# Probabilities of sequences 1 to 3 transposed by VectorE blocks and DMAs through DRAM instead of TensorE, with new engine orders

## The reference

```python
# 1. attention with a sliding window of 64 (4 sequences, 8 heads, head size 64)
scores = scale * q @ k.T ; scores where not (0 <= i - j < 64) = -1e9
attn = exp(scores - max) ; attn = attn / (sum(attn) + 1e-9)
x = attn @ v                                  # -> (4, 576, 512)
# 2. gated MLP with a spatial (token) mixing
h = relu(x @ w_in) ; u, v = halves of h       # 512 each
v_s = einsum('ts,bsd->btd', w_spatial, layernorm(v)) + b_spatial
y = (u * v_s) @ w_out
# 3. mixer: over tokens, then over channels
h = relu(y.T @ w_tok1) @ w_tok2 ; u2 = y + h.T
out = u2 + relu(u2 @ w_ch1) @ w_ch2
```

## Time and profile before

| | |
|---|---|
| median of 3 runs | 691.25 us (691.11 to 691.32) |
| profiled execution, its own time | 691.28 us |
| span in the profile | 689.4 us |
| TensorE busy | 670.6 us, 97% of the span |
| TensorE's granted clock, mean | 0.997 |
| VectorE, ScalarE, GpSimd busy | 47%, 33%, 22% of the span |
| DMA engines busy | 29.8% on the one queue that SyncE issues |

### The profile page before, as it was taken

The page is one execution under the profiler, slowest core; times in us unless marked ns, Lnnn a source line. Parts: engine busy times, 40 slices in busy tenths (PEclk is TensorE's granted clock), DMA queues, the critical chain, the costliest instruction groups (busy, mean ns, idle before and its releaser), DMA issues.

```text
span 689.4 us, 11477 instructions
## 1 busy us (share of the span) xinstructions
PE 670.6 (97%) x4133; PEld 621.2 (90%) x4133; DVE 323.7 (47%) x893; ACT 229.5 (33%) x642; POOL 150.8 (22%) x237
## 2 busy tenths in 40 slices
...
DMA packets 139555, 50.66 MB, mean 73 GB/s; under 512 B 124145, under 2 KB 127793, under 8 KB 139505
## 3 DMA queue, kind: packets, MB, share of 16 engines
q1 hardware_dynamic: 139504, 50.00, 29.8%
...
## 4 chain that ended last, share of the span: by engine, by line
PE 92%; DVE 3%; issue 1%; DMA 1%; ACT 1%; POOL 1%; SPq 0%; DVEq 0%; ACTq 0%; POOLq 0%
PE ps L1123 68%; PE ps L1219 11%; PE ps L1188 5%; PE ps L1163 4%; PE ps L1173 2%; DMA att<-in_moe_w_ch_dram 1%; PE ps L1282 1%; DVE gate L1008 1%; PE ps L1142 1%; DVE arena L1014 1%; DVE att L907 0%; ACT att L700 0%; PE ps L1207 0%; DVE att L1111 0%; ACT arena L776 0%
## 5 line engine op out<-in xcount | busy, mean ns | idle before, releaser
L1123 PE MATMUL ps<-arena 128*128 128x288 f32 (+3 forms) x2064 | 354.5, 326 | 5.4 <-DVE att_r L1047 4.3
L1123 PEld LDWEIGHTS ps<-arena 128*128 128x128 f32 (+1 forms) x2064 | 324.8, 187 | 24.4 <-DVE att_r L1047 4.7
L1123 PE MATMUL ps<-arena,att_r 128*128 128x512 f32 x648 | 161.1, 393 | 0.0
L1047 DVE SCALAR_TENSOR_TENSOR att_r<-ps,att_r 128x384 fp32r<-128x384 f32 x72 | 39.9, 556 | 228.7 <-ACT att_r L810 228.7
L1123 PEld LDWEIGHTS ps<-arena,att_r 128*128 128x128 f32 x648 | 120.6, 188 | 22.0
L810 ACT ACTIVATE att_r<-ps 128x384 fp32r<-128x384 f32 x72 | 35.3, 491 | 241.8 <-PE ps L1123 241.8
L1219 PE MATMUL ps<-arena 128*128 128x288 f32 (+1 forms) x560 | 89.8, 316 | 0.0
L638 POOL TENSOR_SCALAR att<-att,rinv 128x128 f32<-128x128 f32 x144 | 55.8, 408 | 135.5 <-DVE rinv L918 135.3
L1219 PEld LDWEIGHTS ps<-arena 128*128 128x128 f32 x560 | 80.3, 188 | 3.9
L720 ACT ACTIVATE att<-att,nmax 128x128 f32<-128x128 f32 x144 | 55.9, 390 | 14.4 <-DVE nmax L907 14.3
L1188 PE MATMUL ps<-att 128*128 128x128 f32 x288 | 37.6, 276 | 3.3 <-DVE att L927 3.1
...
## 6 DMA issues: line engine op xcount, KB each, us to landing
u_scratch<-uy SPq DMA_DIRECT2D x16, 288.0 KB, 2.8
att<-u_rows SPq DMA_DIRECT2D x18, 256.0 KB, 5.0
out_dram<-att SPq DMA_DIRECT2D x18, 256.0 KB, 2.1
att<-in_v_dram SPq DMA_DIRECT2D x16, 256.0 KB, 3.7
att<-in_k_dram SPq DMA_DIRECT2D x48, 72.0 KB, 2.5
att<-in_q_dram SPq DMA_DIRECT2D x48, 72.0 KB, 2.8
u_rows<-early SPq DMA_DIRECT2D x48, 72.0 KB, 2.7
...
```

What stands on the lines that cost most here:

```text
L1047: dve.scalar_tensor_tensor(out=h3[:, j % RING, 1, :], in0=ps[:, 6 + j % 2, 0:CK], scalar=0.0, in1=h3[:, j % RING, 0, :].bitcast(F32), op0= ...
L1123: ins = pe.matmul(dst, w[a], x[c], start=first and n == 0, stop=last and n == 2, skip_group_check=True)
```

## The change

For sequences 1 to 3 the 27 `T` units of TensorE and the 27 `c` units of VectorE are gone. In their place VectorE turns the probabilities in 32 x 32 blocks from `prob` to `pT` (`pt`), in an order that makes a block-row of all four head pairs contiguous; one DMA (`pw`) stores the 256 KB to a scratch tensor in DRAM, and four DMAs (`pr`) of 64 KB bring them back with the block-rows and block-columns exchanged, into the same buffer `pT`. `V` then reads its moving operand as four pieces of 32 columns, 128 columns apart. Sequence 0 keeps the old way. `m` of a block waits for `pt` of three blocks earlier. `pt` waits for `V` of two blocks earlier. All lists of orders are new; those of POOL and the ACT and DVE lists of the earlier segments are left out below.

```diff
     FIRST_PE = (
-        "g00 + g10 + S0 S1 g20 + g30 + g01 + g11 + g21 + g31 S2 T0 S3 + y00 + y10 + y20 + y30 + y01 S4 V0 S5 T1 "
-        "t0 + y11 + T2 V1 t1 y21 + y31 + S6 T3 V2 a0 a1 t2 T4 V3 t3 S7 V4 t4 a2 a3 a4 T5 S8 T6 V5 v0 + V6 T7 b00 "
-        "b10 b20 b30 b01 b11 b21 b31 v1 V7 T8 + V8 v2 + v3 + v4 + u00 + u10 + u20 + u30 + u01 + u11 + u21 + u31 +").split()
+        "g00 + g10 + S0 S1 g20 + S2 g30 + g01 + g11 S3 + g21 + g31 + y00 + y10 + V0 S4 y20 V1 S5 + y30 + y01 + "
+        "y11 + y21 S6 V2 t0 t1 S7 + y31 + a0 V3 t2 a1 t3 V4 S8 t4 a2 a3 v0 a4 + V5 V6 b00 v1 + b10 b20 v2 + b30 "
+        "V7 V8 b01 b11 b21 b31 v3 + v4 + u00 + u10 + u20 + u30 + u01 + u11 + u21 + u31 +").split()
     LOOP_PE = (
-        "g00 S0 S1 + g10 + g20 + g30 + g01 + g11 + S2 T0 S3 T1 g21 + g31 V0 S4 S5 + y00 + y10 + T2 S6 V1 V2 y20 + "
-        "y30 + y01 + t0 T3 t1 T4 y11 + y21 + y31 + V3 S7 t2 T5 V4 t3 S8 t4 T6 V5 a0 a1 a2 a3 T7 a4 V6 V7 v0 + b00 "
-        "T8 b10 b20 V8 b30 v1 + b01 b11 b21 v2 + b31 v3 + v4 + u00 + u10 + u20 + u30 + u01 + u11 + u21 + u31 +").split()
+        "S0 S1 g00 + g10 S2 S3 + g20 + g30 + g01 + g11 + g21 + g31 + y00 + V0 S4 V1 S5 y10 + y20 + y30 + y01 + "
+        "y11 V2 t0 S6 V3 + y21 + y31 + S7 t1 t2 S8 V4 t3 t4 a0 a1 a2 a3 v0 a4 V5 V6 + v1 + b00 b10 b20 b30 b01 "
+        "b11 V7 V8 v2 + b21 b31 v3 + v4 + u00 + u10 + u20 + u30 + u01 + u11 + u21 + u31 +").split()
...
     LOOP_DVE = (
...
+        "qt0 qt1 qt2 m0 qt3 m1 qt4 r0 r1 m2 pt0 sa00 sm00 pt1 gl00 sa10 sm10 sa20 qt5 m3 sm20 gl10 sa30 gl20 sm30 "
+        "sa01 r2 gl30 sa11 sm01 r3 sm11 pt2 m4 gl01 pt3 sa21 gl11 sm21 sa31 sm31 gl21 vo1 gl31 r4 m5 qt6 pt4 r5 "
+        "m6 qt7 vo2 tl0 pt5 qt8 r6 tl1 tl2 vo3 pt6 m7 tl3 m8 r7 tl4 r8 al0 pt7 al1 pt8 vo4 te00 te10 vs0 te20 "
+        "te30 vs1 vn0 vl0 te01 te11 vn1 te21 te31 vl1 vs2 kt0 ut0 ut1 vn2 vs3 vl2 ut2 vs4 vn3 vn4 ut3 vl3 kt1 vl4").split()
...
     EPILOGUE_ACT = (
-        "gh00 gh10 gh20 wb0 gh30 wb1 gh01 wb2 gh11 wb3 yy00 gh21 wb4 gh31 yy10 wb5 yy20 wb6 yy30 yy01 th0 yy11 "
-        "th1 yy21 wb7 yy31 uf0 th2 wb8 th3 th4 ah0 ah1 wb9 H0 H1 wb10 wb11 wb12 wb13").split()
+        "wb0 gh00 wb1 wb2 gh10 gh20 gh30 gh01 gh11 wb3 gh21 gh31 yy00 yy10 yy20 wb4 yy30 wb5 yy01 th0 th1 yy11 "
+        "wb6 yy21 wb7 yy31 uf0 th2 th3 wb8 th4 ah0 ah1 wb9 wb10 wb11 H0 wb12 wb13 H1").split()
...
     ALL_SP = (
...
+        "lq00 lk00 lq01 lv00 lv01 lq02 lk01 lk02 lw00 lw01 lk03 lq03 lw02 lv02 lv03 lz04 lw04 lv04 lk10 lw06 lq10 "
+        "lw03 pw10 lv10 pw11 pr10 pr11 lw05 lv11 pw12 pw13 pr12 lv12 pr13 pw14 pr14 pw15 lv13 pw16 pr15 pr16 lv14 "
+        "pw17 pw18 pr17 pr18 lk20 st00 st01 st02 st03 lq20 sr00 sr01 sr02 sr03 pw20 pr20 pw21 lv20 lv21 pr21 pw22 "
+        "pw23 pr22 pr23 lv22 pw24 pr24 pw25 lv23 pw26 pr25 pr26 lv24 pw27 pw28 pr27 pr28 lk30 st10 st11 st12 st13 "
+        "lq30 sr10 sr11 sr12 sr13 pw30 pw31 pr30 pr31 lv30 pw32 lv31 pw33 pr32 pr33 lv32 pw34 pr34 pw35 lv33 pw36 "
+        "pr35 pr36 pw37 lv34 pw38 pr37 pr38 wb40 st20 sr20 st21 st22 sr21 st23 sr22 sr23 wb41 wb42 wb43 wb44 wb45 "
+        "wb46 wb47 uf40 wb48 wb49 wb410 wb411 wb412 wb413 st30 st31 sr30 sr31 sr32 sr33 st32 st33").split()
...
+        prob_dram = nc.dram_tensor("prob_blocks", (2, 4, P, P), F32, kind="Internal").ap()
...
+        def back_count(g):
+
+            return sum(n % 2 == g % 2 for n in range(BL, g + 1))
...
+                if kind == "pw":
+                    g = BL * b + x
+                    sp.wait_ge(prob_turned, PROB_TURNED["pt", b, x])
+                    sp.dma_start(prob_dram[g % 2].rearrange("j q n -> q j n"), pT[:, g % 2, :].rearrange("q (j n) -> q j n", j=4)) \
+                        .then_inc(prob_out_dram[g % 2], 16)
+                if kind == "pr":
+                    g = BL * b + x
+                    sp.wait_ge(prob_out_dram[g % 2], 16 * back_count(g))
+                    for j in range(4):
+                        sp.dma_start(pT[32 * j:32 * j + 32, g % 2, :].rearrange("c (i n) -> c i n", i=4),
+                                     prob_dram[g % 2, j].rearrange("(i c) n -> c i n", c=32)).then_inc(prob_back[g % 2], 16)
...
-                    dve.wait_ge(*use_full("T", b0, blk0))
+                    dve.wait_ge(*(use_full("T", b0, blk0) if b0 == 0 else (prob_turned, PROB_TURNED["pt", b0, blk0])))
...
+            def turn_prob(b, blk):
+
+                g = BL * b + blk
+                b0, blk0 = divmod(g - 2, BL)
+                dve.wait_ge(*use_full("V", b0, blk0))
+                apart(dve)
+                dve.wait_ge(prob_done, g + 1)
+                dve.transpose(pT[:, g % 2, :].rearrange("q (j p r) -> q p j r", j=4, p=PAIRS),
+                              prob[:, g % 3, :].rearrange("q (p j r) -> q p j r", p=PAIRS, j=4)).then_inc(prob_turned, 1)
...
-                pe.wait_ge(*use_free("T", b, blk))
+                if b == 0:
+                    pe.wait_ge(*use_free("T", b, blk))
+                    keys = pT[:, g % 2, :].rearrange("k (p n) -> k p n", p=PAIRS)
+                else:
+                    pe.wait_ge(prob_back[g % 2], 64 * back_count(g))
+                    keys = pT[:, g % 2, :].rearrange("k (i p r) -> k p i r", i=4, p=PAIRS)
                 for p in range(PAIRS):
                     ins = pe.matmul(tp[:, bank, P * p:P * (p + 1)], window[:, P * p:P * (p + 1)],
-                                    pT[:, g % 2, P * p:P * (p + 1)], start=True, stop=True)
+                                    keys[:, p], start=True, stop=True)
```

More of the change, by code:

```diff
@@ L57, in bass_attention_gmlp_mixer_kernel @@
     PROLOGUE_PE = (
-        "Q0 K0 Q1 S0 K1 S1 S2 K2 S3 Q2 T0 V0 S4 T1 S5 V1 T2 T3 V2 V3 T4 v0 T5 V4 V5 Q3 + K3 v1 + Z4 S6 S7 v2 S8 "
-        "w0 + u00 + u10 + T6 u20 T7 V6 w1 + T8 V7 u30 V8 w2 + v3 w3 w4 + v4 + u01 w5 + u11 + u21 + u31 +").split()
+        "Q0 K0 Q1 S0 S1 K1 K2 S2 Q2 S3 T0 T1 S4 V0 T2 V1 T3 K3 Q3 S5 V2 S6 V3 T4 w0 v0 w1 w2 V4 S7 T5 Z4 w3 + V5 "
+        "v1 + S8 T6 v2 + V6 T7 u00 w4 + u10 + T8 V7 u20 V8 + u30 + v3 + w5 v4 + u01 + u11 + u21 + u31 +").split()
     FIRST_PE = (
-        "g00 + g10 + S0 S1 g20 + g30 + g01 + g11 + g21 + g31 S2 T0 S3 + y00 + y10 + y20 + y30 + y01 S4 V0 S5 T1 "
@@ L68, in bass_attention_gmlp_mixer_kernel @@
+        "b11 V7 V8 v2 + b21 b31 v3 + v4 + u00 + u10 + u20 + u30 + u01 + u11 + u21 + u31 +").split()
     EPILOGUE_PE = (
-        "g00 + g10 + g20 + g30 + g01 + g11 + g21 + g31 + y00 + y10 + y20 + y30 + y01 + y11 + t0 t1 y21 + y31 + a0 "
-        "t2 a1 t3 t4 a2 a3 a4 H0 H1 b00 b10 b20 b30 b01 b11 b21 b31").split()
+        "g00 + g10 + g20 + g30 + g01 + g11 + g21 + g31 + y00 + y10 + y20 + y30 + y01 t0 t1 + y11 + y21 + y31 + a0 "
+        "t2 t3 a1 t4 a2 a3 a4 H0 b00 b10 b20 b30 b01 b11 b21 b31 H1").split()
@@ L71, in bass_attention_gmlp_mixer_kernel @@
     PROLOGUE_ACT = (
[L72 to L73 removed]
+        "qe0 qe1 e0 e1 qe2 e2 e3 o0 o1 e4 qe3 xh0 o2 e5 wh0 o3 wh1 xh1 o4 e6 vr0 o5 ze4 xh2 e7 wh2 vh0 vr1 wh3 e8 "
+        "wh4 o6 uu00 vr2 o7 xh3 o8 xh4 uu10 uu20 vh1 uu30 vr3 vh2 vr4 wh5 uu01 vh3 vh4 uu11 uu21 uu31").split()
     FIRST_ACT = (
[L75 removed]
@@ L76, in bass_attention_gmlp_mixer_kernel @@
-        "e5 o2 yy31 th2 e6 th3 th4 o3 e7 o4 ah0 ah1 o5 vr0 o6 e8 o7 vr1 vh0 o8 vr2 vh1 vh2 vr3 uu00 vr4 uu10 uu20 "
-        "vh3 vh4 uu30 uu01 uu11 uu21 uu31").split()
+        "gh00 e0 e1 gh10 gh20 e2 gh30 gh01 e3 gh11 o0 yy00 yy10 o1 gh21 gh31 yy20 e4 yy30 yy01 yy11 e5 th0 th1 "
+        "yy21 e6 yy31 th2 o2 th3 o3 th4 e7 e8 o4 ah0 ah1 vr0 o5 vr1 vh0 o6 o7 vr2 vh1 o8 vr3 vh2 vr4 uu00 uu10 "
+        "vh3 uu20 vh4 uu30 uu01 uu11 uu21 uu31").split()
     LOOP_ACT = (
-        "gh00 e0 gh10 e1 gh20 gh30 e2 e3 gh01 o0 e4 yy00 gh11 o1 gh21 o2 gh31 yy10 yy20 yy30 e5 yy01 th0 th1 yy11 "
@@ L80, in bass_attention_gmlp_mixer_kernel @@
-        "yy21 e6 yy31 o3 th2 o4 th3 th4 e7 e8 o5 ah0 ah1 o6 o7 vr0 o8 vr1 vh0 vh1 vr2 vh2 vr3 uu00 uu10 vr4 vh3 "
-        "uu20 vh4 uu30 uu01 uu11 uu21 uu31").split()
+        "e0 e1 gh00 e2 gh10 gh20 e3 gh30 yy00 o0 gh01 gh11 e4 yy10 gh21 gh31 yy20 yy30 o1 yy01 e5 th0 yy11 e6 "
+        "yy21 yy31 o2 th1 th2 th3 o3 th4 e7 e8 o4 ah0 ah1 o5 vr0 vr1 o6 o7 vh0 o8 vh1 vr2 vr3 vh2 vr4 uu00 uu10 "
+        "vh3 uu20 uu30 vh4 uu01 uu11 uu21 uu31").split()
     EPILOGUE_ACT = (
-        "gh00 gh10 gh20 wb0 gh30 wb1 gh01 wb2 gh11 wb3 yy00 gh21 wb4 gh31 yy10 wb5 yy20 wb6 yy30 yy01 th0 yy11 "
@@ L88, in bass_attention_gmlp_mixer_kernel @@
-        "wl1 vn2 xl4 wl2 kt1 wl3 vl2 wl4 vs3 vs4 vn3 wl5 vn4 vl3 vl4").split()
+        "ke0 m0 vo1 m1 ke1 r0 ke2 r1 m2 m3 hv0 hv1 r2 c0 c1 r3 m4 c2 hv2 hu0 c3 hu1 ke3 r4 m5 lv0 xl0 hv3 c4 vo2 "
+        "r5 lv2 wl0 m6 c5 m7 xl1 hu2 hu3 r6 wl1 vs0 xl2 vo3 vn0 r7 c6 m8 wl2 wl3 vl0 r8 vs1 c7 vo4 c8 vs2 wl4 xl3 "
+        "vn1 kt0 vn2 xl4 vl1 kt1 vl2 vs3 vs4 wl5 vn3 vn4 vl3 vl4").split()
     FIRST_DVE = (
[4 rows of a table removed]
-        "vs4 ut3 vn4 vl3 vl4 kt1").split()
[4 rows of a table added]
+        "vs4 vn3 ut2 vl3 ut3 vn4 kt0 vl4 kt1").split()
```

22 lines of the change are left out of this document (12 added, 10 removed), and 15 rows, old and new, of tables (ALL_SP, FIRST_DVE, LOOP_DVE).

## The result

| | before | after |
|---|---|---|
| median, run side by side | 691.25 us (691.11 to 691.32, 4 runs) | 671.91 us (671.60 to 672.14, 4 runs) |
| span of the profiled execution | 689.4 us | 670.2 us |

The ratio is 0.971, 95% interval 0.9697 to 0.9723: faster, by 2.9%. First the page of the kernel after, against the earlier trace rows: TensorE does 108 matmuls fewer, is busy 13.4 us less, and is idle for 13.0 us instead of 18.8.

What follows compares the result with a forecast made beforehand. TensorE was taken as the bound, busy 670.6 of 689.4 us. From 691.3, minus 11.9 (transposes), 4.3 (epilogue stall) and 0.5 (gate), plus 2 (`V` waits) and 2 (boundaries), gave 678.6 us, range 672 to 684.

Steps and rivals of the forecast that it cites:

- `T` removed: TensorE in sequences 1 to 3: dropping 27 transpose units of 0.44 us each saves 11.9 us in full.
- epilogue stall: Epilogue: TensorE's 4.28 us idle goes once wb410 to wb413 load ahead of `st30`; minus 4.3 us.
- gate: Epilogue: TensorE's gate wait of 1.1 us may go or grow; minus 0.5 us (minus 1.1 to plus 1.5).
- waits of `V`: Sequences 1 to 3: all waits of `V` together add 2 us (0 to 8).
- trip: `pt`, store to DRAM and reads back: 7.5 us per block, bounds 6.5 and 9.3, fitting everywhere by 1 to 3 us.
- boundaries: Both segment boundaries: q may load late for the next segment's first unit; plus 2 us together (0 to 6).
- prologue: Start of the kernel: same units in another order, still limited by the exponent chain; 0 us (minus 2 to plus 2).
- + 2 + 2: End of the forecast sum: 2 us for all waits of `V` plus 2 us for both segment boundaries.
- Given back: Rival for the whole kernel: the gain was nowhere or is given back exactly; 690 to 692.5 us, chance 0.04.
- slower: Rival: the DRAM round trip becomes the bound, near 702 us at an 11.5 us trip; chance 0.13, DRAM trip 0.10 of it.
- break-even: Sequences 1 to 3: the gain of 16.7 us is lost at a trip of 10.6 us, given mean slack of 1.7 us.
- Plain DMAs are the wrong tool: Rival on the store: if its pieces cost like 128-byte ones, the trip is 9.7 us, time 685; no separate chance.

## Why the prediction was too high

| step | predicted | measured | from |
|---|---|---|---|
| `T` removed, 27 x 0.44 | -11.9 | -11.7 busy; -11.4 with the waits | second stretch |
| epilogue stall | -4.3 | -5.7 | fourth stretch; half clock 1.40 |
| gate | -0.5 | -1.5 | third stretch |
| waits of `V` | +2 | +0.3 | waits; at most 0.6 without the trip |
| boundaries | +2 | 0 | S0 never idle behind q |
| prologue | 0 | -0.4 | first stretch |

All errors but small ones lie on one side. The differences are -1.4 (clock), -1.0 (gate), -1.7 (trip), -2 (boundaries), -0.4 (prologue) and small remainders, together the missing 6.5 us between 678.6 and the profiled 672.1.

**The mechanisms held, the sizes did not.** The transposes were on the bound and are saved in full: taken out, 11.7 us (the new epilogue with and without them); put back, 11.0. The strided operand is free (276 ns), `pt` costs 0.71 for 0.70. The stall came from the four weight loads behind `st30`: moving these alone removed it.

**The step that failed was a size in the sum.** The largest was its last line, "+ 2 + 2": 4 us for waits that the same text had shown to fit, everywhere, by 1 to 3 us. Its own lists gave 8.6 us of need against 9.6 of slot; a forecast of the likeliest case would have put 0 there and kept the 4 us for the upper bound. The measured total is 0.3. The trip was also overestimated, 7.5 against 6.7: I had put the last read at 2.5 us, by the 72 KB DMAs in 128-byte pieces, and the 64 KB ones in 512-byte pieces took 2.0.

**The second was the price of a stall.** I took the idle time, 4.28 us, as the whole cost. The rows in hand said more: 12 matmuls of 128x384 at 3.65 us, and a clock of 0.97 over a stretch with work in it. The removed stall gave back 5.68 us.

**The third was the gate**, "minus 0.5 (minus 1.1 to plus 1.5)": the wait of 1.12 us vanished in full and 0.4 more with it. With the lists of before it is back at 1.1 us, and with only the loads moved it stays, so the four lists make it go; which of their moves does it was not tried apart, and where the last 0.4 come from was not traced.

**The rivals.** *Given back* and *slower* were real mechanisms of this kernel, one edit away: q behind 16 small DMAs gives 692.6 us, eight reads 695.6, two stores 714.5. The break-even in the text, a trip of 10.6 us, was wrong: with eight reads a single block's trip is 0.7 + 2.5 + 3.2 + 1.8 = 8.2 us, and the gain is gone already. It averaged the slack over pairs and counted one block's trip, not the issues of two blocks that pass SyncE one after the other; and it left out the half clock behind some of the waits. So the chance of 0.10 for that rival hung on a threshold that lay too far away: the waits begin where a cycle needs 9.6 us, and this kernel needs 7.7.

*Plain DMAs are the wrong tool*: not so here. The 256 KB store in 512-byte pieces took 2.6 us and a read 2.0, near those of the earlier trace rows. The Trainium skill (VectorE: DVE Perf Modes, "The three transpose paths" and "Rules for kernel authors") prefers TensorE for a tile of 128 x 128. The runs differ, in a kernel bound by TensorE: VectorE plus DRAM has the longer latency, 6.7 us against 0.44 + 0.69, but off the bound it costs 0.3 us.
